# x laid out in memory tile by tile, with the first x block's rounding and low parts moved behind other work

## The reference

```python
# attention, for each chunk of 32 queries: 16 keys to the left, 8 to the right, 8 memory keys
scores = scale * np.matmul(q_c, k_full.transpose(0, 1, 3, 2))
scores = scores - np.max(scores, axis=-1, keepdims=True)
a = np.exp(scores)
a = a / (np.sum(a, axis=-1, keepdims=True) + 1e-09)
out[:, :, c_start:c_end] = np.matmul(a, v_full)
...
# first MLP: h = x @ w_in (2048 wide), a rational function of h, then @ w_out
P = a[0] + a[1] * h + a[2] * h2 + a[3] * h3
Q = 1.0 + np.abs(b[0]) * np.abs(h) + np.abs(b[1]) * h2
g = P / (Q + 1e-06)
...
# second MLP
a = x @ w1
b = x @ w2
h = a * b @ w3
return (h @ w_out).astype(np.float32)
```

## Time and profile before

| | |
|---|---|
| median of 3 runs | 1119.52 us (1117.95 to 1120.29) |
| profiled execution, its own time | 1119.28 us |
| its span, first to last instruction | 1117.5 us |
| TensorE busy | 1083.3 us (97%) |
| VectorE busy | 712.3 us (64%) |
| ScalarE busy | 582.6 us (52%) |
| GpSimd busy | 169.3 us (15%) |
| mean granted TensorE clock | 0.994 |

### The profile page before, as it was taken

The page is one execution under the profiler, slowest core; times in us unless marked ns, Lnnn a source line. Parts: engine busy times, 40 slices in busy tenths (PEclk is TensorE's granted clock), DMA queues, the critical chain, the costliest instruction groups (busy, mean ns, idle before and its releaser), DMA issues.

```text
span 1117.5 us, 16467 instructions
## 1 busy us (share of the span) xinstructions
PE 1083.3 (97%) x6292; PEld 891.6 (80%) x6292; DVE 712.3 (64%) x995; ACT 582.6 (52%) x960; POOL 169.3 (15%) x136
## 2 busy tenths in 40 slices
PE   7999887998999999999999999999999999999998
PEld 6877775876888888888888888888888888888886
DVE  5279967999999999999998998811112121111211
ACT  4457765766777877867787787512213122221311
POOL 4424543234012122122100100100000000000000
PEclk9999988999999999999999999999999999999999
DMA  9989996112211211120100146320202010020001
GB/s 298 254 220 251 278 253 169 38 39 76 84 56 47 84 56 47 65 76 28 56 38 0 38 151 226 113 76 1 76 0 75 0 38 38 0 75 0 38 1 38
DMA packets 138733, 97.65 MB, mean 87 GB/s; under 512 B 89548, under 2 KB 118220, under 8 KB 137676
## 3 DMA queue, kind: packets, MB, share of 16 engines
q1 hardware_dynamic: 126028, 90.92, 26.7%
q10 hardware_dynamic: 12672, 6.29, 1.9%
HBM read 65.74 MB, written 31.46 MB: 87 GB/s over the span
## 4 chain that ended last, share of the span: by engine, by line
PE 60%; DVE 28%; issue 6%; ACT 4%; DMA 1%; ACTq 1%; SPq 0%; DVEq 0%
PE banks L1236 23%; PE banks L1251 11%; PE banks L1220 9%; PE banks L214 8%; DVE nr L1134 5%; DVE nr L1131 5%; PE banks L711 4%; DVE nr L1138 4%; DVE sq L1114 4%; DVE g_lo L1143 3%; DVE poly L1121 3%; PE banks L730 1%; PE banks L758 1%; DVE poly L1124 1%; DVE probs L642 1%
## 5 line engine op out<-in xcount | busy, mean ns | idle before, releaser
L1220 PE MATMUL banks<-g_hi,weights 128*128 128x512 f32 x768 | 252.4, 390 | 4.5 <-DVE g_lo L1143 4.3
L214 PE MATMUL banks<-x_hi,weights 128*128 128x512 f32 x768 | 251.7, 390 | 0.0
L1236 PE MATMUL banks<-x_hi,weights 128*128 128x512 f32 x768 | 244.2, 389 | 0.0
L1175 DVE TENSOR_TENSOR nr<-habs,banks 128x512 f32<-128x512 f32 x48 | 33.0, 688 | 256.7 <-ACT habs L1066 256.7
L1220 PEld LDWEIGHTS banks<-g_hi,weights 128*128 128x128 f32 x768 | 144.1, 188 | 37.6 <-DVE g_lo L1143 7.4
L1236 PEld LDWEIGHTS banks<-x_hi,weights 128*128 128x128 f32 x768 | 144.1, 188 | 30.0
L214 PEld LDWEIGHTS banks<-x_hi,weights 128*128 128x128 f32 x768 | 144.2, 188 | 29.9
L1066 ACT ACTIVATE habs<-banks 128x512 f32<-128x512 f32 x48 | 28.6, 596 | 245.2 <-PE banks L1236 245.2
L1220 PE MATMUL banks<-g_lo,weights 128*128 128x512 f32 x384 | 149.5, 389 | 0.0
L214 PE MATMUL banks<-x_lo,weights 128*128 128x512 f32 x384 | 149.4, 389 | 0.0
L1236 PE MATMUL banks<-x_lo,weights 128*128 128x512 f32 x384 | 149.4, 389 | 0.0
(11 more groups left out here) (82 smaller groups left out, 1546.8 us busy)
## 6 DMA issues: line engine op xcount, KB each, us to landing
x_raw<-x_transposed_dram SPq DMA_DIRECT2D x12, 1024.0 KB, 5.3
weights<-second_mlp_weights_dram SPq DMA_DIRECT2D x8, 1536.0 KB, 6.3
second_mlp_weights_dram<-split SPq DMA_DIRECT2D x16, 512.0 KB, 3.0
v_sb<-in_v SPq DMA_DIRECT2D x44, 160.0 KB
qk_sb<-in_q SPq DMA_DIRECT2D x24, 256.0 KB, 4.5
x_transposed_dram<-xt_sb ACTq DMA_DIRECT2D x24, 256.0 KB, 4.4
x_transposed_dram<-y_sb SPq DMA_DIRECT2D x6, 1024.0 KB, 4.9
out<-y_sb SPq DMA_DIRECT2D x5, 1024.0 KB, 4.2
```

Source lines behind the costliest of these rows:

```text
L214: last = nc.tensor.matmul(to[:, :], slot[:, m, a, cols], x[:, c, :], start=c == 0 and n == 0, stop=c == KC - 1 and n == 2)
L1220: last = nc.tensor.matmul(bank[4 + c][:, :], slot[:, m, a, cols], g[:, m % G_BUFS, :], start=m == 0 and n == 0, stop=m == SLOTS - 1 and n ...
L1236: last = nc.tensor.matmul(bank[2 * (j % 2) + w][:, :], bslot[:, j, 2 + 2 * w + a, cols], x[:, c, :], start=c == 0 and n == 0, stop=c == KC ...
```

## The change

In memory, each partition's x is laid out by tiles: first the tile of 128 tokens, then the four chunks, then the tokens. A store of one tile is then one run of 2 KB a partition in place of four runs of 512 bytes, and a load of one block is one run of 8 KB a partition in place of four of 2 KB. `x_raw` has the same order, so that the instructions that read a chunk of it (`x_his`, `x_los`, `x_lo_odd`) read four runs of 128 elements. The first MLP's result takes the same form: `copy_y` is replaced by `copy_x2`, which writes four runs of 128 elements, for all blocks of the first MLP. In tiles 18 and 19 ScalarE does `x_his` at the end of the tile's step, and VectorE does `x_los` behind tiles 19 and 20.

```diff
-        self.x_raw = place("x_raw", [P, KC, BLK])
+        self.x_raw = place("x_raw", [P, BLK // P, KC, P])
+        self.x_next = self.y_sb[:, :, :].rearrange("p a b -> p (a b)").rearrange("p (t k c) -> p t k c", t=BLK // P, k=KC)
...
+def by_tile(ap):
+
+    return ap.rearrange("p k t -> p (k t)").rearrange("p (t c) -> p t c", c=DM)
+
+
+def in_tiles(ap):
+
+    return ap.rearrange("p (t c) -> p t c", c=P)
...
-                sp.dma_start(x_raw[:, :, :], xT[:, :, 0:BLK]).then_inc(x_loaded, 16)
+                sp.dma_start(x_raw[:, :, :, :].rearrange("p t k c -> p t (k c)"), by_tile(xT)[:, 0:BLK // P, :]).then_inc(x_loaded, 16)
...
-            act.dma_start(xT[:, :, bass.ds(b * S + pos * P, P)], xt_sb[:, pos % 2, :, :])\
+            act.dma_start(by_tile(xT)[:, bass.ds(b * TPB + pos, 1), :],
+                         xt_sb[:, pos % 2, :, :].rearrange("p a c -> p (a c)").unsqueeze(1))\
...
-                nc.scalar.activation(x_hi[:, c, :], x_raw[:, c, :], ACT.Copy).then_inc(x_hi_ready, 1)
+                nc.scalar.activation(in_tiles(x_hi[:, c, :]), x_raw[:, :, c, :], ACT.Copy).then_inc(x_hi_ready, 1)
...
             copy_pT(b, pos)
-            if last and pos == 0:
-                act.wait_ge(x_loaded, 16)
-                act.wait_ge(turned, 1 + TURNED * (2 * B - 1))
-            if last and pos < 2:
-                x_his(range(2 * pos, 2 * pos + 2))
...
             store_x(b, pos)
+            if last and pos == 0:
+                act.wait_ge(x_loaded, 16)
+                act.wait_ge(turned, 1 + TURNED * (2 * B - 1))
+            if last and pos < 2:
+                x_his(range(2 * pos, 2 * pos + 2))
...
-            if t in (TILES - 6, TILES - 5):
-                x_los(2 * (t - TILES + 6))
+            if t in (TILES - 5, TILES - 4):
+                x_los(2 * (t - TILES + 5))
...
+        def copy_x2(n):
+
+            act.wait_ge(y_stored, n * 16 + 16)
+            for c in range(KC):
+                act.wait_ge(y_done, n * KC + c + 1)
+                nc.scalar.activation(sh.x_next[:, :, c, :], in_tiles(bank[4 + c][:, :]), ACT.Copy).then_inc(y_act, 1)
...
             if y_before is not None:
-                copy_y(y_before)
+                copy_x2(y_before)
...
-        copy_y(NBLK - 1)
+        copy_x2(NBLK - 1)
```

More of the change, by code:

```diff
@@ L451, in x_lo_odd @@
             pool.wait_ge(x_hi_ready, c + 1)
-            pool.tensor_tensor(out=x_lo[:, c, :], in0=x_raw[:, c, :], in1=f32(x_hi[:, c, :]),
+            pool.tensor_tensor(out=in_tiles(x_lo[:, c, :]), in0=x_raw[:, :, c, :], in1=in_tiles(f32(x_hi[:, c, :])),
                                op=ALU.subtract).then_inc(sh.x_lo_pool, 1)
@@ L683, in x_los @@
             dve.wait_ge(x_hi_ready, c + 1)
-            nc.vector.tensor_tensor(out=x_lo[:, c, :], in0=x_raw[:, c, :], in1=f32(x_hi[:, c, :]),
+            nc.vector.tensor_tensor(out=in_tiles(x_lo[:, c, :]), in0=x_raw[:, :, c, :], in1=in_tiles(f32(x_hi[:, c, :])),
                                     op=ALU.subtract).then_inc(sh.x_lo_dve, 1)
@@ L889, in load @@
         def load(src, i):
-            sp.dma_start(x_raw[:, :, :], src[:, :, bass.ds(i * BLK, BLK)]).then_inc(x_loaded, 16)
+            sp.dma_start(x_raw[:, :, :, :].rearrange("p t k c -> p t (k c)"),
+                         by_tile(src)[:, bass.ds(i * (BLK // P), BLK // P), :]).then_inc(x_loaded, 16)
         def store_x2(i):
             sp.wait_ge(y_act, i * KC + KC)
-            sp.dma_start(x2T[:, :, bass.ds(i * BLK, BLK)], y_sb[:, :, :]).then_inc(y_stored, 16)
+            sp.dma_start(by_tile(x2T)[:, bass.ds(i * (BLK // P), BLK // P), :],
+                         sh.x_next.rearrange("p t k c -> p t (k c)")).then_inc(y_stored, 16)
         def store_out(i):
```

## The result

| | before | with the change |
|---|---|---|
| median of 5 runs | 1119.88 us | 1114.85 us |
| lowest to highest | 1117.95 to 1120.58 | 1112.50 to 1116.76 |
| profiled execution | 1119.28 us | 1112.50 us |
| span | 1117.5 us | 1110.7 us |

The ratio is 0.996 with an interval of 0.9942 to 0.9979: 2.4 to 6.5 us less. The forecast was 1115.0. In a later group of runs two executions of the kernel before took 6175 us, which nothing here explains; the ratios leave them out.

What follows compares the result with a forecast made beforehand. TensorE is busy 97%, so gains lie in its gaps: VectorE paces attention, and at 160 to 180 engines wait for each other. 1119.28 - 3.7 (moved low parts) - 0.6 (layout) = 1115.0 us; 8 in 10: 1111.5 to 1118.3.

Steps and rivals of the forecast that it cites:

- The moved low parts: Last batch of attention: moving x_his and x_los later cuts VectorE's waits from 8.3 to about 4 us, gaining 3.7 us.
- the walk: Step-by-step rebuilding of the changed order in tiles 18 to 21: tile 21 ends at 181.4 in place of 185.16.
- The product with v ends at 168.51: TensorE, tile 18: end time from the old trace; copy of x follows at 169.2, first rounding ready at about 170.5.
- is covered by 1.4 us: ScalarE's copy_pT of tile 19, queued behind the roundings: product with v until 172.2, needed only at 174.8.
- The layout: Stores of 128 packets in place of 512, up to the transfer at 155.81: 0.6 us gained, between nothing and 1.9.
- I take a third: Of at most 1.9 us from 16 cheaper stores, 0.6 us was counted, as VectorE sets the pace in most tiles.
- Rival 1: Product with v at 155.81 loses its 1.78 us wait and the low clock behind: up to 4.9 us more, 1110.7; chance 0.15.
- Rival 2: TensorE's clock falls over the MLP's first products: up to 3 us of the 3.7 lost, 1118.5; chance 0.15.
- Rival 3: Start-up per run of 128 lengthens low parts and copies at five block ends: 7 us, 1122.0, slower; chance 0.04.
- Rival 4: First x_hi comes 3.5 us later, at 174, so VectorE's new waits equal the old: time 1119; chance 0.06.
- needs an x block that lands after 173: Condition given for VectorE's waits staying as long: the first x block lands after 173 in place of 163.7.

Runs made afterwards that it cites:

- the repeat: The changed kernel run again with not a line changed, in 12 more runs: median 1115.69 us, ratio 0.9965 against the kernel before.

## Why the prediction was right, and where it wasn't

**The moved low parts: right in kind, and in size within the noise.** The sum had 3.7 us for them; the moves alone gave 4.8 with an interval of 3.0 to 6.6 (1119.2 times 0.0027 to 0.0059). From the end of tile 18 to the end of tile 21 the walk had 18.7 us, and the changed kernel's first trace has 18.0. The two waits ahead of the low parts, 8.3 us before, were to be about 4 and were 3.4 there. The first was taken as 2.5 and was 3.17: `total` of tile 19 did not wait for the exponential, where the walk had 1 us, so VectorE came to the low part sooner. The second was taken as 1.5 and was 0.25: `normalise` of tile 20 took 1.75 us, 0.8 more than the walk had, and the rounding came 0.4 us sooner behind `centre`. One sum of the walk is off by a little: the six instructions of a tile take 4.0 us by the rows named, not 3.9.

**A step that holds in one trace only: "The product with v ends at 168.51".** The walk took TensorE's product of tile 18 from the trace of before, 5.8 us behind the end of tile 18. In the changed kernel's first trace it is 5.2 us, in that of the moves alone 6.7, in the repeat's 8.6, with waits for v of 1.58, 3.27 and 4.34 us. The moves don't bring that: nothing that was moved stands ahead of this product, and in the trace of the layout alone it waits too (2.34 us, 6.5 behind tile 18). What the moves bring is who pays. As ScalarE's rounding now stands behind the copy of x, which waits for that product, the lateness reaches VectorE. The sentence that the queue behind the moved instructions "is covered by 1.4 us" looked at what stands behind the roundings; what they stand behind was the place to look. The roundings behind the exponential cut that path: the wait ahead of the first low part is 0.23 us and less, even where the product waits 2.22 us.

**The layout: the term was mis-sized.** It was taken as 0.6 us of a possible 1.9, and is nothing that 12 runs can tell (-1.8 to +1.3 us). The saving in engine time was right (2.1 engine-us a store where 2.0 was forecast). The step that failed is the one from engine time to path, "I take a third". That VectorE sets the pace in those tiles would explain it, but no run tests that; transfers make TensorE wait 6.8 us between 70 and 200 in the trace of the layout alone, against 2.4 before. For this change the rule of the Trainium skill, "DMA: Bandwidth & Descriptors", section Specifications, gave the better term. On the engine time the measurement differs from it and decides: 19 bytes per ns in 512-byte packets and 22 in those of 2 KB. That 1115.0 came within 0.2 us of the median is luck: by the two experiments 3.7 is low by 1.1 and 0.6 is high by 0.6, both inside the noise.

**Rival 1, the transfer at 155.81, comes in time.** It doesn't: 2.02 us of wait in the first trace. But the stretch at the low clock behind it was absent there. This belongs to the 2.4 us by which the profiled pair is apart at the end of tile 18. It is absent in the trace of the layout alone too, and in that of the kernel before with v ahead, and neither median falls; so it isn't a gain of the change. The runs of one kernel spread over 7 us, and where the clock falls and which transfer is late differ from trace to trace.

**Rival 2, the clock takes the gain back.** It was low at 173.01 (1.94 us for eight transposes) and high again at 178.49 (1.08), before the first product of the MLP. Out for this trace. But it happens: in four of the fourteen traces the first product itself takes 0.58 or 0.78 us in place of 0.48, the repeat's at 185.15 among them. From its start to the end these take 933.8 to 934.6 us, and the other ten 933.0 to 933.3, so it costs 0.5 to 1.6 us and not up to 3.

**Rival 3, the four runs cost.** Out: in the first MLP VectorE's low part takes 1.78 us beside GpSimd's as before, and the copies on the chain 1.95 for four. Alone, VectorE's low parts take 0.69 and 0.78 us in the layout alone, 0.69 and 0.77 in the kernel before with v ahead. **Rival 4, the waits are only moved,** is true of single executions and not of the median. The repeat's trace has it (7.8 us of waits), with the x block landed at 165.9. That it "needs an x block that lands after 173" was wrong: a late product with v does it too.

## What to carry to other kernels

An instruction that is moved later on its engine inherits the waits of all it is put behind, so put it behind what its reader needs anyway (here the exponential) and no further. A load that is in time in one trace can be late in the next: before blaming a change for a wait, look whether the wait stands in front of everything that was changed, and whether it is there without the change. Compare a stretch between two fixed points and not only the ends of two traces. Fewer and larger packets made the stores cheaper for the DMA engines here and won no time.

## What was not expected of the hardware

The clock doesn't fall in the same place each time: behind a wait of 1.78 us the product with v ran at 1.97 us, behind one of 2.02 us at 1.15 in the changed kernel, whose order on TensorE is the same up to there. The issue of a store on ScalarE took 0.35 us for 128 runs of 2 KB in place of 0.55 for 512 runs of 512 bytes, and the layout alone won nothing. And with v ahead of q and k only two products wait for v in six traces (100 to 195 us), some of the waits stand at q and k instead, and by itself the order had 0.9999 on the kernel before.
